# Attention with units that mix two heads: transposes in one group, other engines for copies and roundings

## What is computed

```python
scores = scale * np.matmul(q, k.transpose(0, 1, 3, 2))
bias = slopes[:, None, None] * (-np.abs(rel).astype(np.float32))[None, :, :]
mask = (rel >= 0) & (rel < window)
scores = np.where(mask, scores + bias[None], -1000000000.0)
scores = scores - np.max(scores, axis=-1, keepdims=True)
attn = np.exp(scores)
attn = attn / (np.sum(attn, axis=-1, keepdims=True) + 1e-09)
attn_out = np.matmul(attn, v)
x = np.ascontiguousarray(attn_out.transpose(0, 2, 1, 3)).reshape(B * S, H * D)
h = np.maximum(x @ w_in, 0.0);  x = h * h @ w_out       # first layer
h = x @ w_in;  out = h * np.cos(h) @ w_out              # second layer
```

## Time and profile before

| | us |
|---|---|
| median of 3 runs | 853.29 (853.18 to 854.99) |
| the profiled execution, own time | 853.7 |
| its span | 851.8 |
| PE busy in the span | 843.3 (99%) |
| DVE busy | 648.1 (76%) |
| ACT busy | 522.7 (61%) |
| POOL busy, all of it in attention | 79.4 (9%) |

### The profile page before, as it was taken

How to read it: one execution, slowest core, us unless ns; L and a number is a source line. 1 busy time by engine, 2 the same in 40 slices (tenths; PEclk the granted TensorE clock), 3 DMA queues, 4 the chain that set the end, 5 groups by cost and what they waited for, 6 DMA issues and landing times.

```text
span 851.8 us, 16172 instructions
## 1 busy us (share of the span) xinstructions
PE 843.3 (99%) x5846; PEld 766.7 (90%) x5846; DVE 648.1 (76%) x1456; ACT 522.7 (61%) x1145; POOL 79.4 (9%) x174
## 2 busy tenths in 40 slices
PE   7999999999999999999999999999999999999998
PEld 5888999999999999999999998999899889899996
DVE  7999979787687676696776787767887777767665
ACT  7999444342353343343433787777787777787775
POOL 7779500000000000000000000000000000000000
PEclk9999999999999999999999999999999999999999
DMA  7775716647588788679768556556575655675522
GB/s 244 235 245 187 274 68 254 209 161 258 204 294 306 247 283 313 243 259 322 266 239 303 192 192 195 180 188 197 171 257 191 190 191 174 206 244 176 192 74 75
DMA packets 72190, 185.34 MB, mean 218 GB/s; under 512 B 7216, under 2 KB 19760, under 8 KB 70064
## 3 DMA queue, kind: packets, MB, share of 16 engines
q1 hardware_dynamic: 71248, 183.23, 63.9%
q10 hardware_dynamic: 864, 1.08, 0.4%
HBM read 141.82 MB, written 42.47 MB: 216 GB/s over the span
## 4 chain that ended last, share of the span: by engine, by line
PE 97%; DVE 2%; ACT 0%; issue 0%; POOL 0%; DVEq 0%
PE psum L697 41%; PE psum L731 23%; PE psum L736 15%; PE psum L738 8%; PE psum L635 4%; PE psum L593 3%; PE psum L538 2%; PE psum L547 0%; ACT probs L827 0%; PE psum L555 0%; DVE hidden_sum L1241 0%; DVE work L1290 0%; DVE probs L1114 0%; DVE g_lo L1295 0%; POOL probs L512 0%
## 5 line engine op out<-in xcount | busy, mean ns | idle before, releaser
L697 PE MATMUL psum<-xt_hi,comb 128*128 128x384 f32 x1344 | 381.6, 336 | 0.2
L697 PEld LDWEIGHTS psum<-xt_hi,comb 128*128 128x128 f32 x1344 | 246.5, 188 | 10.6 <-DVE hidden_sum L1241 0.4
L731 PE MATMUL psum<-wout,g_hi 128*128 128x512 f32 x576 | 178.4, 391 | 0.0
L1295 DVE TENSOR_TENSOR g_lo<-work,g_hi 128x384 fp32r<-128x384 f32 x192 | 102.5, 553 | 73.9 <-ACT g_hi L928 72.5
L736 PE MATMUL psum<-g_hi,wout 128*128 128x512 f32 x384 | 148.9, 391 | 0.0
L928 ACT ACTIVATE g_hi<-work 128x384 fp32r<-128x384 f32 x192 | 97.5, 519 | 69.0 <-DVE work L1290 41.1
L697 PE MATMUL psum<-x_lo,comb 128*128 128x384 f32 x384 | 128.6, 335 | 0.0
L731 PEld LDWEIGHTS psum<-wout,g_hi 128*128 128x128 f32 x576 | 107.2, 188 | 19.0
L731 PE MATMUL psum<-wout,g_lo 128*128 128x512 f32 x288 | 113.2, 393 | 0.0
L738 PE MATMUL psum<-g_hi,wout 128*128 128x256 f32 x384 | 107.5, 280 | 0.0
L840 ACT ACTIVATE part_a<-psum 128x384 f32<-128x384 f32 x48 | 23.6, 491 | 126.4 <-PE psum L697 126.4
(11 more groups left out here) (94 smaller groups left out, 1273.0 us busy)
## 6 DMA issues: line engine op xcount, KB each, us to landing
comb<-comb SPq DMA_DIRECT2D x80, 768.0 KB, 5.6
wout<-wout SPq DMA_DIRECT2D x48, 512.0 KB, 3.3
comb<-comb SPq DMA_DIRECT2D x8, 1792.0 KB, 6.9
comb<-kept SPq DMA_DIRECT2D x8, 1792.0 KB, 6.9
wout_raw<-w_out SPq DMA_DIRECT2D x48, 256.0 KB, 5.9
comb<-comb SPq DMA_DIRECT2D x40, 256.0 KB, 3.2
v_raw<-v SPq DMA_DIRECT2D x16, 512.0 KB, 3.4
raw<-w_in SPq DMA_DIRECT2D x32, 256.0 KB, 7.2
```

The costliest lines, as they stand in the source:

```text
L697: last = pe.matmul(psum[:, H_BANK + i % 2, 0:NH], wi, mi[:, k, :], start=first, stop=True, skip_group_check=True)
L731: last = pe.matmul(psum[:, Y_BANK + c, :], g[:, r, tok], w, start=start and m == 0, stop=True, skip_group_check=True)
L1295: dve.tensor_tensor(g_lo[:, r, cols], work[i][:], g_hi[:, r, cols].bitcast(F32), ALU.subtract)\
```

## The change

- **Units mix the heads.** Unit (i, j) holds head j's first 64 queries of a block and the other head's last 64. The order of the score products is the same, their places in the banks change; the bias tables take their scale from a column of `slopes` with one value for each half of the partitions; the tail tables go (the tail uses an ordinary one). In the values, the products of half height come as (lower rows, head 0), (upper, head 1), (lower, head 1), (upper, head 0) instead of (lower, 0), (upper, 1) twice.
- **PE's order.** The tail scores move to the scores of block 3 (edge_scores); all four fills of a pair are transposed together, before the values; fills 2 and 3 use the banks of the edge scores. Waits are changed to match: edge scores wait for ACT's three copies of pair s-3, fill 2 for the bias of the next pair's three edge units.
- **Copies.** ACT copies fill 3 (256 columns) instead of DVE, and the last pair's x.
- **Roundings.** POOL rounds the first weights (768 columns, loop steps 5 and 8), their sums (1024 columns, 6 and 9) and blocks B11, B21, B22 of x (768 columns, 7, 10, 11), each after its normalise. ACT keeps T3, T1, T2 (steps 13, 14, 15, before its fifth exponential) and T4. The order in which xt_hi_ready counts blocks changes with it (FIRST_HI_ORDER). FIRST_LO, POOL's half blocks of low parts, stays as it is.

```diff
-ORDER = [7, 8, 1, 3, 0, 5, 2, 4, 6]
+ORDER = [8, 7, 0, 1, 3, 5, 2, 4, 6]
-EARLY_UNITS = [3, 6, 9, 9]
+EARLY_UNITS = [4, 6, 9, 9]
+EDGE_UNITS = 3
-FIRST_HI = {11: "B11", 12: "T3", 13: "B21", 14: "T2", 15: "B22"}
+FIRST_HI_POOL = {7: "B11", 10: "B21", 11: "B22"}
+FIRST_HI_ACT = {13: "T3", 14: "T1", 15: "T2"}
+FIRST_HI_ORDER = [*FIRST_HI_POOL.values(), *FIRST_HI_ACT.values(), "T4"]
 FIRST_LO = {12: ("T3", 0), 13: ("B11", 0), 14: ("B11", 1), 15: ("T3", 1)}
...
+        PT_BANKS = [4, 5, 2, 3]
...
+            def first_weights_hi(n):
+                pool.wait_ge(raw_landed[n], 32)
+                pool.tensor_scalar(comb[:, n, 0, 0:3, :], raw[:, n, 1:4, :], 1.0, 1.0, ALU.mult, ALU.mult)\
+                    .then_inc(comb_hi_ready, 1)
...
             def first_moving_lo(name, k):
                 pool.wait_ge(t_done, T_READ[name])
-                pool.wait_ge(xt_hi_ready, HI_ORDER.index(name) + 1)
+                pool.wait_ge(xt_hi_ready, hi_done(0, name))
...
             for s in range(1, PAIRS + 1):
                 normalise(s - 1)
+                if s in (5, 8):
+                    first_weights_hi(s // 8)
+                elif s in (6, 9):
+                    first_sums_hi(s // 9)
+                elif s in FIRST_HI_POOL:
+                    first_moving_hi(FIRST_HI_POOL[s])
                 if s in FIRST_LO:
                     first_moving_lo(*FIRST_LO[s])
...
-                    last = pe.matmul(score_of(unit_of(i, h))[HALF * half:HALF * half + HALF], q_raw[d, r, q0:q0 + HALF],
+                    last = pe.matmul(score_of(unit_of(i, h ^ half))[HALF * half:HALF * half + HALF], q_raw[d, r, q0:q0 + HALF],
...
-            def first_scores(p):
+            def edge_scores(p):
...
-                    pe.wait_ge(biased, UNITS * (p - 1) + 2)
+                    pe.wait_ge(biased, UNITS * (p - 1) + EDGE_UNITS)
+                if p >= 3:
+                    pe.wait_ge(pt_act, 3 * (p - 2))
                 scores(p, 3).then_inc(scores_ready, 1)
+                tail_scores(p).then_inc(scores_ready, 1)
...
+                if fill == 2:
+                    pe.wait_ge(biased, UNITS * min(p + 2, PAIRS - 1) + EDGE_UNITS)
+                elif fill == 0 and p > 0:
+                    pe.wait_ge(pt_act, 3 * p)
+                elif fill == 1 and p > 0:
+                    pe.wait_ge(pt_dve, p)
...
                 for i in range(1, 4):
-                    for odd in range(2):
-                        n = 2 * i + odd
-                        product(0, n, keys_at(0, HALF * n, lower), REST_AT[i] + HALF * odd, final=n == 7)
-                        block = v_first[upper, r, :] if n == 2 else keys_at(1, HALF * (n - 3), upper)
-                        product(1, n, block, REST_AT[i] + HALF * odd, final=n == 7)
+                    even, odd = 2 * i, 2 * i + 1
+                    product(0, even, keys_at(0, HALF * even, lower), REST_AT[i])
+                    product(1, even, v_first[upper, r, :] if i == 1 else keys_at(1, HALF * (even - 3), upper), REST_AT[i])
+                    product(1, odd, keys_at(1, HALF * odd, lower), REST_AT[i] + HALF, final=i == 3)
+                    product(0, odd, keys_at(0, HALF * (odd - 3), upper), REST_AT[i] + HALF, final=i == 3)
...
             for s in range(PAIRS):
-                first_scores(s)
+                edge_scores(s)
+                other_scores(s)
...
-                other_scores(s)
-                if s > 2:
-                    transposes(s - 2, 0)
                 if s >= 2:
-                    transposes(s - 2, 1)
+                    all_transposes(s - 2)
                 if s >= 3:
                     values(s - 3)
-                if s >= 2:
-                    transposes(s - 2, 2)
-                    transposes(s - 2, 3)
             pe.wait_ge(biased, UNITS * PAIRS)
             hidden_product(0, 0)
             values(PAIRS - 3)
-            transposes(PAIRS - 2, 0)
-            transposes(PAIRS - 2, 1)
+            all_transposes(PAIRS - 2)
             hidden_product(0, 1)
-            transposes(PAIRS - 2, 2)
-            transposes(PAIRS - 2, 3)
             hidden_product(0, 2)
             values(PAIRS - 2)
-            transposes(PAIRS - 1, 0)
-            transposes(PAIRS - 1, 1)
+            all_transposes(PAIRS - 1)
             hidden_product(0, 3)
-            transposes(PAIRS - 1, 2)
-            transposes(PAIRS - 1, 3)
...
             for s in range(PAIRS):
-                if s >= 5:
-                    copy_pt(s - 3, 2)
-                if s in (5, 8):
-                    weights_hi(s // 8)
-                elif s in (6, 9):
-                    sums_hi(s // 9)
-                elif s in FIRST_HI:
-                    round_moving(0, FIRST_HI[s])
                 for n, u in enumerate(ORDER):
...
+                    if n == (0 if s < 4 else 1) and s >= 2:
                         copy_pt(s - 2, 0)
+                    if n == (0 if s == 3 else 2) and s >= 2:
+                        copy_pt(s - 2, 2)
+                        copy_pt(s - 2, 3)
+                    if n == 4 and s in FIRST_HI_ACT:
+                        if s == min(FIRST_HI_ACT):
+                            act.wait_ge(xt_hi_ready, len(FIRST_HI_POOL))
+                        round_moving(0, FIRST_HI_ACT[s])
                     exponent(s, u)
...
             def last_pairs():
 
-                copy_pt(PAIRS - 3, 3)
-                invert_sums(PAIRS - 1)
                 split_moving(0, "B21")
                 split_moving(0, "T1")
+                invert_sums(PAIRS - 1)
...
             for s in range(PAIRS):
-                if s >= 3:
-                    copy_pt(s - 3, 3)
                 for n, u in enumerate(ORDER):
-                    if s >= 1 and n == (2 if s == 1 else 5):
+                    if s >= 1 and n == (5 if s == 2 else 6):
                         invert_sums(s - 1)
-                        if s == 2:
-                            copy_pt(0, 1)
+                    if s == 3 and n in (1, 8):
+                        copy_pt(n // 8, 1)
+                    elif s in (4, 5) and n == 3:
+                        copy_x(s - 4)
                     bias_scores(s, n, u)
-                if s >= 3:
+                if s >= 5:
                     copy_pt(s - 2, 1)
+                    copy_x(s - 3)
                 attention_extra(s)
-                if s >= 3:
-                    copy_x(s - 3)
+                if s == 4:
+                    copy_pt(2, 1)
```

More of the change, by code:

```diff
@@ L499, in bias_tables @@
             def bias_tables(d):
[L500 to L505, removed]
+                for j in (2 * d, 2 * d + 1):
+                    pool.tensor_scalar(bias[:, j, :], distance[:, 0:BAND], slopes[:, j:j + 1], 1.0, ALU.mult, ALU.mult)
+                    last = pool.tensor_scalar(bias_first[:, j, :], distance[:, BAND:BAND + P], slopes[:, j:j + 1], 1.0,
+                                              ALU.mult, ALU.mult)
+                last.then_inc(bias_pool, 1)
             def normalise(p):
@@ L620, in transposes, with all_transposes @@
                 last.then_inc(transposed, 1)
+            def all_transposes(p):
+                for fill in range(4):
+                    transposes(p, fill)
             def values(p):
@@ L645, in values @@
                     for h in range(2):
-                        product(h, n, keys_at(h, 0), MAIN_AT[0][h] + HALF * n, first=True)
-                for i in range(1, 4):
-                    for odd in range(2):
-                        for h in range(2):
-                            product(h, 2 * i + odd, keys_at(h, P * (i - 1) + HALF * (odd + h)), MAIN_AT[i][h] + HALF * odd)
+                        product(h, n, keys_at(h, 0), MAIN_AT[0][h ^ n] + HALF * n, first=True)
+                for n in range(2, 8):
+                    for h in range(2):
+                        i, j = n // 2, h ^ n % 2
+                        product(h, n, keys_at(h, HALF * (n - 2 + j)), MAIN_AT[i][j] + HALF * (n % 2))
                 for h in range(2):
@@ L835, in copy_pt, with copy_last_x @@
                 at, w = FILL_COL[fill], FILL_COLS[fill]
[L836 removed]
+                act.activation(pt[p % 2][:, at:at + w], psum[:, PT_BANKS[fill], 0:w], ACT.Copy).then_inc(pt_act, 1)
+            def copy_last_x():
+                p = PAIRS - 1
+                b, d = divmod(p, H // 2)
+                act.wait_ge(pv_done, p + 1)
+                halves = x[:, d, b * S:b * S + S].rearrange("p (n c) -> p n c", c=HALF)
+                act.activation(halves[:, 0::2, :], psum[:, O_BANK, 0:5 * HALF].rearrange("p (n c) -> p n c", c=HALF), ACT.Copy)
+                act.activation(halves[:, 1::2, :], psum[:, O_BANK + 1, 0:4 * HALF].rearrange("p (n c) -> p n c", c=HALF),
+                               ACT.Copy).then_inc(x_ready, 1)
             def copy_part(n):
@@ L1087, in _ @@
             dve.wait_ge(upper_ready, 1)
-            dve.wait_ge(slopes_ready, 1)
```

(9 more changed lines are left out.)

116 lines of the change are left out of this document (52 added, 64 removed).

## The result

The changed kernel takes 859.98 us (859.47 to 861.11, 6 runs) where the kernel before takes 853.66 (853.18 to 854.99, 6 runs): ratio 1.0075, 95% interval 1.0063 to 1.0088. It is 6.3 us slower. The forecast was 856.2, range 851.8 to 860.5, slower with a chance of 0.63. The sign and the range held; the loss forecast, 2.9 us, is less than half of the 6.3 measured. The profiled execution's own time is 861.11, its span 858.8, 7.0 above that of before.

The account below looks back on a forecast made before the run. PE sets the pace at 5.55 us a step, with three engines close behind. Pair 12's values 3.6 behind, less 1.85, plus 1.2 give +2.9 us: 856.2, range 851.8 to 860.5.

Parts of the forecast that it names:

- PE's own gain: PE's step from 5.55 to 4.86 us: two tile-shape changes gone, 0.34; half-height values as quadruples on four quarters, 0.35.
- R5: Rival: PE gains nothing from quadruples; values 0.35 longer, 0.17 a step in loop and end: 857.5, counted with the forecast.
- R4: Rival: the PSUM bank rule turns score quadruples into pairs, 1.1 us more a step, PE at 6.0: 859 to 862; chance 0.03.
- POOL's prices: Roundings moved to POOL cost 0.81 ns a column: 0.82 us for 768 columns, 1.03 for 1024.
- R3: Rival: POOL's roundings cost double, 860.6 us; chance 0.12.
- Wait (A): Steps 5 and 6: DVE's low parts wait for POOL's roundings; steps take 7.35 and 7.8 instead of 5.55, 4.0 us lost.
- R1: Rival: slack swallows both waits, steps run at 4.96 to 5.0, 2.4 us won, 850.9; chance 0.12.
- R2: Rival: gains and waits cancel, 852 to 855 us, say 853.7; chance 0.25.
- Steps 7 to 11: Loop pace of 5.2 us a step, over ACT's 4.96; steps 7 to 12 were to win 2.0 us.
- The circle of two steps: Each pair's inverse, POOL, transposes, values, x copies, extra and next inverse: 10.4 us over two steps, 5.2 each.
- Wait (B): Step 12: POOL's low half of T3 waits for ACT's step 13 rounding, 3.0 us idle; pair 14 starts at 89.3.
- The end: After pair 12's values: PE wins 1.85 us, but POOL's 12.4 us chain from pair 14 loses 1.2.

Follow-up runs that it names:

- experiment 9: Experiment 3's kernel with odd half-height value products naming the other head, so all fall on two quarters (values partly wrong): 854.66 us, ratio 1.0007.
- experiment 5: Experiment 3's kernel without the guard, the addition of 1e-9 to the sums before DVE's inverse: 851.55 us, ratio 0.9968.
- experiment 1: Changed kernel with POOL's first weights and sums roundings one loop step earlier, behind pairs 3 and 4: 856.15 us, ratio 1.0025.
- experiment 3: Changed kernel with both order moves, first roundings a step earlier and POOL's half blocks as B11, B11, T3, T3: 852.40 us, ratio 0.9982.
- experiment 8: Experiment 3's kernel with one more 768-column rounding on POOL in step 10: 851.55 us, ratio 0.9972.
- experiment 2: Changed kernel with POOL's half blocks in the order B11, B11, T3, T3 instead of T3, B11, B11, T3: 856.08 us, ratio 1.0025.
- experiment 4: Changed kernel with all roundings back on ACT at the start of its steps, PE's new order and ACT's third copy kept: 854.39 us, ratio 1.0005.
- experiment 10: Experiment 3's kernel with four more 768-column roundings on POOL in step 10: 855.14 us, ratio 1.0014.

## Why the prediction was right or wrong

**That the time lies in the range is partly luck.** The range reached up to 860.5 because POOL's roundings might have cost double, and they did not. The 3.8 us beyond the forecast came from other terms, below.

**PE's own gain: right.** Its work in a step is 4.90, forecast 4.86. The quadruples are worth 0.35 a step in the stretch (experiment 9); both changes of shape are gone in the loads above, and by difference they are worth 0.3, which no run shows alone. R5 is out. R4 is out too: the score quadruples of the new layout, whose two row halves write one bank at a time, take 1.72 where they took 1.66, and R4 asked for 1.1 more; the half-height values run on four quarters with both row halves in one bank (28 loads in 0.41, and in 0.75 on two quarters). The bank rule of the Trainium skill (TensorEngine Tiling (Array Packing), Gotcha 1: PSUM Pressure) doesn't hold for these products.

**POOL's prices: right.** 0.83 to 0.85 for 768 columns, forecast 0.82; 1.04 to 1.05 for 1024, forecast 1.03. R3 is out.

**Wait (A): right in place and size.** 7.37 and 7.83 between pairs where 7.35 and 7.8 were forecast; pairs 4, 5 and 6 all come 0.25 later than the forecast's clock had them. Taking it away gave back 3.8 us; 4.0 was forecast for the loss. R1, where DVE's and ACT's slack swallows it, is out: so is R2.

**Steps 7 to 11: the term was too small.** 5.46 a step instead of 5.2: 1.3 us by pair 11. The circle of two steps was the right one. In its sum I took the inverse at 0.34, a row from where POOL was idle. The chain of waits of the changed kernel has it at the place:

```profile
59.83 0.50 DVE guarded L1145
60.32 0.02 issue
60.35 0.23 DVE inverse L1148
60.57 0.08 issue
60.65 0.43 POOL probs L519
```

and DVE's timeline the guard of this pair 9 beside that of pair 8:

```profile
54.47 0.16 DVE L1145 TENSOR_SCALAR guarded<-row_sum 128x9 f32<-128x9 f32 x1
...
59.75 0.56 DVE L1145 TENSOR_SCALAR guarded<-row_sum 128x9 f32<-128x9 f32 x1
```

From the guard's start to POOL's start are 0.90 for pair 9 and 54.97 - 54.47 = 0.50 for pair 8, whose guard meets an idle POOL. So the number was short in two ways. The guard is held up by 0.40 until POOL's rounding ends at 60.28 (1.04 from 59.24). And 0.34 is what the inverse takes in DVE's queue; until POOL starts it is 0.50 even undisturbed, 0.16 more. The circle, 49.71 to 60.65, is 10.94 and not 10.4, and these 0.56 cover the miss. In the next circle, 60.65 to 71.73, the way from guard to POOL is 0.69, held up by 0.19 only, and the normalise takes 4.51 where 4.3 was taken. So of the 1.2 us that the two circles lost, the guard held up is about half; the rest is the undisturbed way and POOL's own time.

I had taken DVE's subtractions as something that holds up POOL, and not seen that the same holds the other way, although the kernel before has it too: where POOL's half blocks of low parts lie ahead of an inverse (steps 12 to 14), it starts the next pair 0.38 after them (pair 14 in the earlier trace rows). The Trainium skill has the rule (SBUF — State Buffer, Who interferes with whom): whichever of a DVE operation in a two-port mode and a GpSimd operation starts first holds the shared ports for its whole length. The trace agrees: the guard ends where POOL's operation ends, and takes 0.35 to 0.56 beside a rounding, 0.17 without one; that it runs in such a mode no row shows. This change puts a rounding on POOL in each step from 5 to 11, just where the inverse falls due, so the rule spoke against it.

That the guard is worth its whole hold-up is not shown: without it (experiment 5) the pace went down by 0.11 a step, because DVE and POOL are both close to the limit and the next of them takes over.

**Wait (B): the idle time right, its price too small.** 3.16 idle, forecast 3.0. From pair 11 to pair 14 the forecast had 89.3 - 70.2 = 19.1; with wait (A) removed (experiment 1) it is 87.98 - 68.68 = 19.3. In the changed kernel it is 92.69 - 71.73 = 20.96. The 1.65 more lie between pairs 13 and 14: 7.40 against 5.74 there. In that stretch TensorE ran at the lower of its two levels, 1.2 GHz:

```profile
84.00:90.60 6.60, 6.19 (x95) 5.47 (x99) 2.34 (x5) 4.73 (x19) 5.79 (x12) 0.50 0.02 8
```

and the same stretch of experiment 1:

```profile
84.00:90.60 6.60, 6.15 (x119) 5.07 (x111) 6.24 (x27) 6.60 (x26) 6.15 (x13) 1.00 0.55 166
```

95 matmuls in 6.19 us of busy time against 119 in 6.15. The runs of the changed kernel bear the price out: the profiled one and one other have a mean clock of 0.994 and take 861.11 and 860.97; the other four have 0.996, some 3.4 us less at half clock, and take 859.47 to 860.09, 1.3 less on average. The sum counted a wait of PE as lost time only, and had no term for what PE is granted behind it.

**The end: right in kind.** POOL's chain from pair 14 to its end was taken at 12.4 and took 105.58 - 92.69 = 12.9.

**The sum of it.** At the end of POOL's work the changed kernel is 7.6 behind, the forecast had 3.7. The 3.9 missing are: 0.25 at the start, 1.3 from the circle of steps 7 to 11 (about half of it the guard held up), 1.85 from pair 11 to 14, nearly all the half clock, and 0.5 at the end. The values of pair 12 start at 92.82, where 89.0 was forecast and 85.39 was before. From POOL's end 0.8 was to be won back and about 0.6 was: the span is 7.0 longer. The median of the times is 6.3 above before; the profiled execution is the longest of its six.

Three sums of the prediction are off by themselves: the parts of wait (B) add up to 2.9 and not 3.0, six steps at 4.96 are 1.4 less and not 1.3, and pair 12 due at 75.4 plus 13.6 is 89.0 and not 89.3. None of them moves the forecast by more than 0.3.

## What to carry over

When work moves to an engine because it has time left, ask who stands and waits for that work, not how long it takes: the two places where another engine's strict order met POOL's new work cost 7.6 us, and moving them by one or two steps (`s in (4, 8)`, `(5, 9)`, T3's halves last) makes the same change 0.18% [0.09, 0.27] faster than the kernel before. A share of 80% busy, as POOL had the earlier trace rows, hides that POOL and DVE hold each other up; read what a small DVE instruction takes beside a POOL one before putting more on POOL. And where the trace shows the clock falling behind a wait of PE, put the wait down at more than its length.

The quickest version here is that of experiment 5, 851.55, ratio 0.9968 [0.9955, 0.9980], which leaves out the addition of 1e-9 to the sums. Its lead over experiment 3 is no larger than what the start of attention varies between profiles, and experiment 8, with a rounding too many, has the same median; both are faster than the kernel before, their order is open.

## What was unexpected

**TensorE at half clock behind a wait.** The granted clock was 0.50 for 3.4 us (36.0 to 39.4 in the changed kernel) behind PE's idle time in wait (A), and for 6.8 us (83.8 to 90.6) behind that in wait (B):

```profile
34.00:36.00 2.00, 0.43 (x4) 0.46 (x5) 2.00 (x12) 1.10 (x4) 0.00 (x0) 1.00 0.81 220
36.00:39.40 3.40, 3.40 (x69) 2.96 (x71) 1.80 (x11) 3.40 (x16) 2.78 (x8) 0.50 0.60 209
```

PE was busy for 0.43 of the 2 us ahead of the first, and for 0.92 of the 3.4 us from 80.0 to 83.4 ahead of the second. The first stretch cost little, as DVE waited for POOL anyway; the second cost 1.65. In experiment 2, which keeps wait (A), a stretch of 3.4 follows it too, and in the profile of experiment 4 one follows the stall (0.51 from 46.2 to 49.6). But not every wait brings one, not even in the same kernel. The profiled run of experiment 1 keeps wait (B), with PE idle for 2.32 (2.33 in the changed kernel), at full clock, while eight of its ten runs show a mean clock of 0.997 or 0.998, the amount of one short stretch, and are 0.7 to 1.9 us longer than its fastest. PE's wait of 2.5 in experiment 10 was followed by none in the profiled run, and by one in six of the eleven, as far as the mean clock tells. What decides stays open.

**The start of attention varies.** Pair 0's normalise starts at 10.1 to 11.5 in the twelve profiles. A difference of under 1 us between two variants is better read from pair 0 on than from their medians.
